# Twelve pairs of first-layer products share their last pass as two 64-row tiles

## What is computed

```
w   = softmax(weight_gen over its 7 taps)
c   = causal 7-tap convolution of x, one set of taps for each token and head (24 features a head)
h   = c @ w_in                                   # 192 -> 2048
P   = a0 + a1 h + a2 h^2 + a3 h^3
Q   = 1 + |b0| |h| + |b1| h^2
y1  = (P / (Q + 1e-6)) @ w_out                   # 2048 -> 192
xn  = y1 / sqrt(mean(y1^2) + 1e-6) * rms_g
y   = (silu(xn @ w_gate) * (xn @ w_val)) @ w2_out  # 192 -> 1536 -> 192
```

## Time and profile before

| | |
|---|---|
| Median of 3 executions | 1444.98 us (1443.11 to 1447.46) |
| Profiled execution | 1445.34 us, span of its instructions 1443.5 us |
| TensorE matmuls busy | 95% (7040 instructions) |
| VectorE busy | 86% |
| ScalarE busy | 74% |
| GpSimd busy | 32% |
| Mean granted TensorE clock | 0.983 of full |
| DMA | mean 22 GB/s, 32.30 MB |

### The profile page before, as it was taken

How to read it: one execution, slowest core, us unless ns; L and a number is a source line. 1 busy time by engine, 2 the same in 40 slices (tenths; PEclk the granted TensorE clock), 3 DMA queues, 4 the chain that set the end, 5 groups by cost and what they waited for, 6 DMA issues and landing times.

```text
span 1443.5 us, 20421 instructions
## 1 busy us (share of the span) xinstructions
PE 1368.5 (95%) x7040; PEld 1221.0 (85%) x7040; DVE 1247.1 (86%) x1524; ACT 1071.0 (74%) x1387; POOL 458.4 (32%) x283
## 2 busy tenths in 40 slices
PE   2676999999999999999999999999999999999999
PEld 2465898888898888889898888989888898998988
DVE  6999998989889898988989899898989989888621
ACT  4676877878787787888778788877878787777521
POOL 2935240434324143432414343241434314200000
PEclk9788999999999999999999999999999999999999
DMA  8200001000000100000010000001000000000000
GB/s 232 82 0 31 1 2 41 1 32 11 30 11 0 41 0 30 11 30 11 0 41 0 30 11 30 11 0 41 0 30 11 30 12 0 12 0 1 12 12 11
DMA packets 12514, 32.30 MB, mean 22 GB/s; under 512 B 1604, under 2 KB 7234, under 8 KB 12480
## 3 DMA queue, kind: packets, MB, share of 16 engines
q1 hardware_dynamic: 11744, 31.61, 6.8%
q10 hardware_dynamic: 736, 0.23, 0.1%
HBM read 25.55 MB, written 6.29 MB: 22 GB/s over the span
## 4 chain that ended last, share of the span: by engine, by line
PE 76%; DVE 11%; ACT 7%; issue 4%; DMA 2%; SPq 0%; ACTq 0%; POOL 0%; DVEq 0%; POOLq 0%
PE dn L681 32%; PE bank L672 9%; PE bank L673 8%; PE bank L674 8%; PE bank L675 8%; PE bank L676 8%; DVE den L607 4%; ACT seed L484 2%; PE bank L688 2%; DVE num L599 2%; DVE num L596 1%; DVE num L612 1%; DVE num L618 1%; ACT L484 1%; DMA glu<-in_moe_w_val_dram 1%
## 5 line engine op out<-in xcount | busy, mean ns | idle before, releaser
L681 PE MATMUL dn<-dn_w,num 128*128 128x192 f32 x2048 | 378.8, 329 | 17.1 <-DVE num L618 9.9
L681 PEld LDWEIGHTS dn<-dn_w,num 128*128 128x128 f32 x2048 | 343.5, 192 | 24.3 <-DVE num L618 8.6
L469 ACT ACTIVATE den<-bank,coef 128x512 f32<-128x512 f32 x256 | 175.5, 686 | 175.8 <-PE bank L676 164.6
L681 PE MATMUL dn<-dn_w,glu 128*128 128x192 f32 x1536 | 280.8, 327 | 5.3 <-DVE glu L643 5.3
L681 PEld LDWEIGHTS dn<-dn_w,glu 128*128 128x128 f32 x1536 | 254.3, 190 | 12.9 <-DVE glu L643 8.9
L596 DVE TENSOR_TENSOR num<-num,bank 128x512 f32<-128x512 f32 x256 | 173.9, 679 | 70.1 <-ACT num L471 68.1
L612 DVE SCALAR_TENSOR_TENSOR num<-num,coef,seed 128x1024 f32<-128x1024 f32 x128 | 183.5, 1435 | 40.8 <-ACT seed L490 40.3
L471 ACT ACTIVATE num<-bank,coef 128x512 f32<-128x512 f32 x256 | 199.5, 779 | 0.0
L618 DVE SCALAR_TENSOR_TENSOR num<-den,num 128x1024 f32<-128x1024 f32 x128 | 193.1, 1510 | 0.0
L597 DVE SCALAR_TENSOR_TENSOR den<-den,coef,bank 128x512 f32<-128x512 f32 x256 | 188.9, 738 | 0.0
L599 DVE SCALAR_TENSOR_TENSOR num<-num,coef,bank 128x512 f32<-128x512 f32 x256 | 188.9, 738 | 0.0
(11 more groups left out here) (86 smaller groups left out, 1983.4 us busy)
## 6 DMA issues: line engine op xcount, KB each, us to landing
x_in<-in_x_dram SPq DMA_DIRECT2D x14, 960.0 KB
out_dram<-y_out SPq DMA_DIRECT2D x16, 384.0 KB, 2.3
w_blk<-in_weight_gen_dram SPq DMA_DIRECT2D x14, 112.0 KB, 2.0
dn_w<-in_moe_w_out_dram SPq DMA_DIRECT2D x1, 1536.0 KB, 20.7
dn_w<-in_moe_w_out_dram SPq DMA_DIRECT2D x1, 1152.0 KB, 10.6
num<-in_moe_w_in_dram SPq DMA_DIRECT2D x1, 768.0 KB, 6.6
num<-in_moe_w_in_dram SPq DMA_DIRECT2D x2, 384.0 KB, 8.2
seed<-in_moe_w_gate_dram SPq DMA_DIRECT2D x1, 768.0 KB, 10.0
```

What stands on the lines that cost most here:

```text
L681: done = pe.matmul(banks[:, j // 2, j % 2 * D:(j % 2 + 1) * D], acts[:, j * P:(j + 1) * P], w, start=first and j % 2 == 0, stop=last, skip ...
```

## The change

In twelve places of the TensorE order where two first-layer products stand next to each other, the last pass (the one with the weights' low part of the last 64 features) is no longer run by each product alone. The first product of a pair stops after four passes. The second runs its four passes, and then both last passes are issued one after the other as products with 64 contraction rows: the first product's with partitions 0 to 63 of `bl` and `x_b`, the second product's with partitions 64 to 127 of `bl` and of a new tile. In the built program these two have the tile sizes 64x128 at the row positions 0 and 64; all the others stay 128x128 at position 0. There are 12 pairs a block, so 192 pairs in all. For these 24 of the 40 products of a block the cross product of the weights' low part with the low part of the last features is left out.

Partitions 64 to 127 of `x_b` hold the low part, so a second copy of the high part is needed there: `x_bh` and `xn_bh`, of which only partitions 64 to 127 are used. ScalarE writes it from the transposed bank, in one more 64x512 instruction ahead of the one that writes `x_b`, once a block for each. To make room in SBUF the tile `square` goes: the squares that nobody reads are written to `xn_t`, with one wait more for the transposes that read it last.

```diff
+SECOND_OF = {
+    ("up1", 2): ("up1", 1), ("gate", 5): ("value", 3), ("gate", 7): ("value", 6), ("gate", 8): ("value", 7),
+    ("up1", 9): ("up1", 8), ("value", 8): ("gate", 10), ("gate", 11): ("value", 9), ("value", 11): ("value", 10),
+    ("up1", 13): ("up1", 12), ("up1", 15): ("up1", 14), ("gate", 1): ("gate", 0), ("gate", 2): ("value", 0),
+}
+FIRST_OF = {first: second for second, first in SECOND_OF.items()}
...
+        x_bh, xn_bh = sb("x_bh", [P, T], F32R), sb("xn_bh", [P, T], F32R)
...
-        square = sb("square", [P, SLOTS, D])
...
+                if part == 1:
+                    act.activation(x_bh[DB:P, :], bank[XPOSE_BANK[1]][DB:P, :], ACT.Copy).then_inc(xt_hi, 1)
                 act.activation((x_ah, x_b)[part][:, :], bank[XPOSE_BANK[part]][:, :], ACT.Copy).then_inc(xt_hi, 1)
...
+                wait(act, xnt_ready, blk * 2)
                 for j in range(SLOTS):
-                    last = act.activation(square[:, j, :], dn1[:, j // 2, j % 2 * D:(j % 2 + 1) * D], ACT.Square,
+                    last = act.activation(xn_t[:, j, 0:D], dn1[:, j // 2, j % 2 * D:(j % 2 + 1) * D], ACT.Square,
...
+                if part == 1:
+                    act.activation(xn_bh[DB:P, :], bank[XNX_BANK[1]][DB:P, :], ACT.Copy, scale=G_B[DB:P, :]).then_inc(xn_hi, 1)
...
-                wait(dve, xt_hi, blk * 2 + (part + 1))
+                wait(dve, xt_hi, blk * 3 + (1, 3)[part])
...
-                wait(dve, xn_hi, blk * 2 + (part + 1))
+                wait(dve, xn_hi, blk * 3 + (1, 3)[part])
...
+                pe.matmul(out_bank[:, :], bh[:, f], m_b[:, :], start=False, stop=False)
+                if (name, n) in FIRST_OF:
+                    return
+                if (name, n) in SECOND_OF:
+                    lower, k = SECOND_OF[name, n]
+                    lower_banks, lower_ready, _, _, _, lower_bl = FIRST[lower][0:6]
+                    pe.matmul(bank[lower_banks[k]][:, :], lower_bl[0:DB, k * P:(k + 1) * P], m_b[0:DB, :], start=False, stop=True)\
+                        .then_inc(lower_ready, 1)
+                    pe.matmul(out_bank[:, :], bl[DB:P, f], m_bh[DB:P, :], start=False, stop=True).then_inc(ready, 1)
+                else:
+                    pe.matmul(out_bank[:, :], bl[:, f], m_b[:, :], start=False, stop=True).then_inc(ready, 1)
```

More of the change, by code:

```diff
@@ L668, in bank_read, with first_layer @@
                     wait(pe, read, blk * often + (n + 1))
[L670 to L676, removed]
+            FIRST = {"up1": (UP1_BANK, h_ready, up1_ah, up1_al, up1_bh, up1_bl, x_ah, x_al, x_b, x_bh),
+                     "gate": (GATE_BANK, g_ready, up2_ah[:, 0, :], up2_al[:, 0, :], up2_bh[:, 0, :], up2_bl[:, 0, :],
+                              xn_ah, xn_al, xn_b, xn_bh),
+                     "value": (VALUE_BANK, v_ready, up2_ah[:, 1, :], up2_al[:, 1, :], up2_bh[:, 1, :], up2_bl[:, 1, :],
+                               xn_ah, xn_al, xn_b, xn_bh)}
+            def first_layer(name, n):
+                banks, ready, ah, al, bh, bl, m_ah, m_al, m_b, m_bh = FIRST[name]
+                out_bank, f = bank[banks[n]], slice(n * P, (n + 1) * P)
+                pe.matmul(out_bank[:, :], ah[:, f], m_ah[:, :], start=True, stop=False)
+                pe.matmul(out_bank[:, :], ah[:, f], m_al[:, :], start=False, stop=False)
+                pe.matmul(out_bank[:, :], al[:, f], m_ah[:, :], start=False, stop=False)
+                pe.matmul(out_bank[:, :], bh[:, f], m_b[:, :], start=False, stop=False)
[9 more added lines that the diff above has]
+                    pe.matmul(out_bank[:, :], bl[:, f], m_b[:, :], start=False, stop=True).then_inc(ready, 1)
             def second_layer(banks, acts, w, first, last):
@@ L704, in up1 @@
                 bank_read(blk, "up1", c)
-                f = slice(c * P, (c + 1) * P)
-                first_layer(bank[UP1_BANK[c]], up1_ah[:, f], up1_al[:, f], up1_bh[:, f], up1_bl[:, f],
-                            x_ah, x_al, x_b).then_inc(h_ready, 1)
+                first_layer("up1", c)
             def down1(blk, c):
@@ L727, in gate @@
                 bank_read(blk, "gate", m)
-                f = slice(m * P, (m + 1) * P)
-                first_layer(bank[GATE_BANK[m]], up2_ah[:, 0, f], up2_al[:, 0, f], up2_bh[:, 0, f], up2_bl[:, 0, f],
-                            xn_ah, xn_al, xn_b).then_inc(g_ready, 1)
+                first_layer("gate", m)
             def value(blk, m):
@@ L737, in value @@
                 bank_read(blk, "value", m)
-                f = slice(m * P, (m + 1) * P)
-                first_layer(bank[VALUE_BANK[m]], up2_ah[:, 1, f], up2_al[:, 1, f], up2_bh[:, 1, f], up2_bl[:, 1, f],
-                            xn_ah, xn_al, xn_b).then_inc(v_ready, 1)
+                first_layer("value", m)
             def down2(blk, m):
```

## The result

| | before | after |
|---|---|---|
| Median | 1445.95 us (1443.11 to 1447.46, 4 runs) | 1508.54 us (1505.93 to 1510.33, 4 runs) |
| Ratio to before | | 1.044, 95% interval 1.0428 to 1.0452 |
| Span of the profiled execution | 1443.5 us | 1504.1 us |
| One period | 84.58 us | 88.2 or 89.5 us |

What follows compares the result with a forecast made beforehand. TensorE was taken as nearly full, without time to spare at down2 2 and gate 9. Lateness 0.73 - 0.23 = +0.5 us a period, times 13, minus 3 at the edges, gave 1448 us; own range 1438 to 1458, overall 1428 to 1482.

Steps and rivals of the forecast that it cites:

- The wait that I foresaw at down2 2: TensorE would wait some 4 us a period, above all at gate 9 for glu 7 and down2 2 for glu 2.
- I take the saving of a whole slot: At each pair on TensorE: nine slots instead of ten, loads hidden under a pass, 0.227 us saved.
- rival D: At each pair: changing tile form empties the array, costing up to 0.56 us; 1470 to 1492 us; chance 0.22.
- (a): At value 6 with gate 7: late value 6 delays glu 6 and glu 7; gate 9's start slips 0.65 us.
- (b): From gate 9 to linear 12: up1 12 waits for up1 13, ScalarE has no cover, +0.2 us.
- (c): On ScalarE between linear 12 and silu 0: the extra copy x_bh adds 0.5 us, bounds 0 to 0.6.
- the tiles overlapping (1448): The author's main case for the whole kernel: each pair saves a slot, yet +0.5 us a period; 1448 us, chance 0.40.

Runs made afterwards that it cites:

- copies: The changed kernel with no pairs: every product runs five full passes, the extra ScalarE copies and the squares in xn_t stay; 1438.03 us.
- fours: The changed kernel without the pair value 6, gate 7, with three groups of four products running their last passes as two tile pairs in a row; 1515.88 us.
- defer12: The changed kernel with all 12 pairs still deferred, but each last pass a full 128-row one, so no 64-row tiles; 1451.94 us.
- late_inverse: The kernel before with one VectorE step moved: newton 5 stands ahead of the softmax's inverse; 1435.88 us.

## Why the prediction was wrong, point by point

- **The view of what bounds the kernel** held. TensorE nearly full, down2 2 and gate 9 the two places without time to spare: TensorE waited 0.45 at down2 2 before and 1.80 at gate 9 after, and at other places only in the kernel with four products held. The wait that I foresaw at down2 2 after the change did not come. The kernels without a wait put its work at 83.84 a period; I had 83.5.
- **"I take the saving of a whole slot: ... two loads of 0.12 still fit under one pass of 0.227."** This is the step that failed. The two tiles did overlap (0.01 us), as taken, but their loads were not issued under the pass of another form, nor the next full load under theirs. The row of 711.23 that I argued from shows a load ahead of its matmul within one form, and says nothing of a change of form. Measured: 0.41 a pair (0.09 until the pass before is through and 0.11 of load, twice), where my rival D had 0.56; I gave D 0.22. The Trainium skill (TensorEngine Tiling (Array Packing), Tiling Modes, Key Properties) states that a change of the tiling mode drains TensorE. The traces agree: with the lone tile, too, the loads wait at each change, and 0.40 us go.
- **D's own time, 1470 to 1492,** held for the cost of the form by itself: with the lateness moved away the kernel measures 1472.84. That is partly luck, for two errors offset each other. D's price a pair was too high, and it let only five pairs pay. Once a pair costs TensorE time instead of giving it, TensorE is the bound all round and all twelve pay: 83.84 + 2.2 = 86.0. The other 36 us, which carry the result out of D's times too, are the next two points.
- **(a) value 6 with gate 7, 0.65 us at gate 9.** Right place, right mechanism, wrong size: the wait and what goes with it are 2.05 us a period. I let GpSimd's add slip behind qy 1; in the run it came 0.03 us ahead of it, because the way into the tile form, which I had put at nothing, made qy 1 later by another 0.20. Deferred without tiles the add came 0.16 us behind, and the wait was 0.60, near my 0.65.
- **The clock** was in no case of mine. A wait of 1.80 us inside the dense run was followed by passes at the 1.2 GHz level in 5 of 12 periods, 1.3 to 1.5 us each time. With the wait gone, or at 0.60 us, the clock was 1.00 in all these periods. The wait alone does not decide it: behind the 1.81 us of the kernel with four products held the clock fell in one period of eleven. What else does stays open.
- **(b) and (c), +0.5 us for x_bh and +0.2 for up1 12.** The copy was priced nearly right (0.6 us from x_bh's start to x_b's in the kernel of the copies) and its effect had the wrong sign: it delays silu 0, glu 0 and the inverse as I wrote, and that delay let py 6 in ahead of GpSimd's second product: -0.74 us a period. I had taken the 2.66 and 2.86 of the two steps as fixed durations on the chain; part of them was waiting for what both engines share. Deferral of the other eleven pairs costs 84.14 - 83.84 = 0.3 a period, of the order of the 0.2 that I had for up1 12.
- **The forecast** for the tiles overlapping (1448) has no run that answers to it, since the cost of the form can't be taken out.

## What to carry to other kernels

A 64-row tile between 128-row passes costs two changes of form; count 0.4 us for 128x512 passes in fp32r against 0.23 saved by a pair, before asking whether the tiles overlap. Tile pairs that follow each other share one change. When work is held back to be shared, ask who reads the first result and what stands behind that reader: here one deferred product of forty cost 36 to 40 us beside the tiles (9 without them), and moving the reader in its engine's order gave it back. And a long VectorE row beside GpSimd work may be a matter of who came first: move the step that starts GpSimd, and measure.

## What the runs showed of the hardware

- A load of weights ran ahead of its matmul by a slot within one tile form, the 128-row one (705.54 for the pass of 705.76) and the 64-row one (702.66 for 702.88 in fours). At a change of form (128-row to 64-row, or back) it started only 0.09 us after the pass before was through. A pass of 96 rows behaved as one of 128 and cost 0.3% in all (1.0017 to 1.0037).
- Two 64-row tiles at row positions 0 and 64, writing to two banks, start 0.01 us apart and take one slot between them: the next load begins 0.42 us behind them, which is 0.11 of load, a slot of 0.227 and 0.09.
- A VectorE instruction of 128x1024 with two inputs in SBUF takes 1.22 us (newton, qy) or 1.28 (py) in most rows and up to 2.89 when GpSimd's tensor_tensor of 128x768 had begun first. Between 300 and 1200 us of the traces of before, after, defer12, copies and late_inverse it took over 1.35 us 250 times, and each time it ended 1.08 to 1.09 us after one of GpSimd's. At gate 9 a start 0.03 us behind GpSimd's gave 2.89, one 0.16 us ahead of it 1.22. What exactly the two engines share was not tested by itself. GpSimd's pow took 1.02 us where it is recorded 0.06 to 0.09 us ahead of VectorE's qy 1 and 2.10 where it is recorded 0.01 to 0.02 ahead; qy 1 took 1.22 both times.
- TensorE idle for 1.80 us was followed by the 1.2 GHz level in 5 periods of 12 and by none in the other 7, at the same place of the program; at another place, idle for 1.81, in 1 period of 11.
